# Attention over channels and two expert layers: order of the norms and scores, the product for the merged weights, and weight buffers of the second layer

## The reference

```python
qn = q / (norm(q, axis=1) + 1e-06)        # norms run over the 6016 rows, for each channel
kn = k / (norm(k, axis=1) + 1e-06)
s = kn.transpose(0, 2, 1) @ qn / tau      # 256 x 256
a = exp(s - s.max(-1)); a /= a.sum(-1) + 1e-09
x = v @ a                                 # 6016 x 256
h = x @ moe_w_in                          # 256 x 2048
y = (moe_s * relu(h)**2 + moe_b) @ moe_w_out
h = y @ moe2_w_in
out = (max(h, 0) + moe2_alpha * min(h, 0)) @ moe2_w_out
```

## Time and profile before

| | |
|---|---|
| median of 3 runs | 1071.3 us (1070.34 to 1072.33) |
| the profiled execution | 1070.1 us, span 1068.3 us |
| PE busy | 1032.1 us (97% of the span), 4579 matrix instructions |
| DVE busy | 856.6 us (80%) |
| ACT busy | 607.5 us (57%) |
| POOL busy | 40.9 us (4%) |
| chain that ended last | PE 88%, DVE 4%, DMA 2%, SP's queue 2% |
| moved by DMA | 77.04 MB, mean 72 GB/s |
| mean granted clock of PE | 0.985 of full |

### The profile page before, as it was taken

The page is one execution under the profiler, slowest core; times in us unless marked ns, Lnnn a source line. Parts: engine busy times, 40 slices in busy tenths (PEclk is TensorE's granted clock), DMA queues, the critical chain, the costliest instruction groups (busy, mean ns, idle before and its releaser), DMA issues.

```text
span 1068.3 us, 13360 instructions
## 1 busy us (share of the span) xinstructions
PE 1032.1 (97%) x4579; PEld 862.8 (81%) x4579; DVE 856.6 (80%) x1308; ACT 607.5 (57%) x1014; POOL 40.9 (4%) x61
## 2 busy tenths in 40 slices
PE   8879999999999999999979999999999999999995
PEld 6757888888888888888967788888888888888994
DVE  5888998888788798798879978778777777877874
ACT  5565666566567567566656545445445455455452
POOL 1101100000000000020041000000000000000000
PEclk9988999999999999999989999999999999999998
DMA  9721111310410410510740434104104103100201
GB/s 352 236 43 30 40 21 45 114 20 22 137 20 3 156 18 1 164 31 1 264 122 10 146 114 148 30 1 148 30 1 148 31 1 127 34 1 2 38 1 34
DMA packets 136228, 77.04 MB, mean 72 GB/s; under 512 B 102608, under 2 KB 114912, under 8 KB 135904
## 3 DMA queue, kind: packets, MB, share of 16 engines
q1 hardware_dynamic: 136032, 76.18, 23.9%
q0 software_dynamic: 128, 0.01, 0.0%
HBM read 48.44 MB, written 27.72 MB: 71 GB/s over the span
## 4 chain that ended last, share of the span: by engine, by line
PE 88%; DVE 4%; DMA 2%; SPq 2%; issue 1%; ACT 1%; POOL 0%; DVEq 0%; ACTq 0%
PE acc L428 15%; PE acc L430 15%; PE acc L429 15%; PE hab L428 8%; PE hab L429 8%; PE hab L430 8%; PE hcd L428 6%; PE hcd L430 6%; PE hcd L429 6%; PE acc L500 2%; SPq L301 1%; DMA stage<-in_moe_w_in_dram 1%; DMA qk_raw<-in_k_dram 1%; SPq L316 1%; DVE cb L836 1%
## 5 line engine op out<-in xcount | busy, mean ns | idle before, releaser
L653 ACT ACTIVATE g_hi<-cb 128x512 fp32r<-128x512 f32 (+1 forms) x384 | 233.6, 620 | 237.6 <-DVE cb L851 132.6
L428 PE MATMUL acc<-g_hi,wo_hi 128*128 128x512 f32 (+1 forms) x768 | 296.5, 386 | 0.3 <-DVE g_lo L857 0.3
L429 PE MATMUL acc<-g_lo,wo_hi 128*128 128x512 f32 (+1 forms) x768 | 296.2, 386 | 0.0
L430 PE MATMUL acc<-g_hi,wo_lo 128*128 128x512 f32 (+1 forms) x768 | 296.1, 386 | 0.0
L857 DVE TENSOR_TENSOR g_lo<-cb,g_hi 128x512 fp32r<-128x512 f32 (+1 forms) x384 | 245.3, 679 | 54.0 <-ACT g_hi L653 53.1
L428 PEld LDWEIGHTS acc<-g_hi,wo_hi 128*128 128x128 f32 x768 | 144.4, 188 | 27.6 <-DVE g_lo L857 0.6
L429 PEld LDWEIGHTS acc<-g_lo,wo_hi 128*128 128x128 f32 x768 | 144.5, 188 | 27.1
L430 PEld LDWEIGHTS acc<-g_hi,wo_lo 128*128 128x128 f32 x768 | 144.4, 188 | 27.1
L428 PE MATMUL hab<-x_hi,ws_hi 128*128 128x512 f32 (+1 forms) x384 | 149.5, 389 | 11.3 <-ACT u L635 10.5
L851 DVE SCALAR_TENSOR_TENSOR cb<-cb,alph 128x512 f32<-128x512 f32 (+1 forms) x192 | 142.1, 740 | 20.3 <-ACT cb L635 14.2
L429 PE MATMUL hab<-x_lo,ws_hi 128*128 128x512 f32 (+1 forms) x384 | 148.6, 387 | 0.0
(11 more groups left out here) (121 smaller groups left out, 950.0 us busy)
## 6 DMA issues: line engine op xcount, KB each, us to landing
x_dram<-x_hi SPq DMA_DIRECT2D x35, 256.0 KB, 2.6
x_dram<-x_lo SPq DMA_DIRECT2D x35, 256.0 KB, 2.8
x_hi<-x_dram SPq DMA_DIRECT2D x35, 256.0 KB, 4.8
x_lo<-x_dram SPq DMA_DIRECT2D x35, 256.0 KB, 5.1
qk_raw<-in_q_dram SPq DMA_DIRECT2D x10, 512.0 KB, 10.3
qk_raw<-in_k_dram SPq DMA_DIRECT2D x10, 512.0 KB, 11.5
v_raw<-in_v_dram SPq DMA_DIRECT2D x40, 128.0 KB, 3.3
out_dram<-y_sq SPq DMA_DIRECT2D x80, 64.0 KB, 2.2
```

What stands on the lines that cost most here:

```text
L428: pe.matmul(dst, w_hi, m_hi, start=start, stop=False, skip_group_check=True)
L429: pe.matmul(dst, w_hi, m_lo, start=False, stop=False, skip_group_check=True)
L430: return pe.matmul(dst, w_lo, m_hi, start=False, stop=stop, skip_group_check=True)
L653: sc.activation(g_hi[:, blk, 0:w], cb[:, blk, 0:w], ACT.Copy).then_inc(g_hi_done[blk], 1)
```

## The change

- Chunks of q and k are 1, 2, 2, 3, nine times 4, 2, 1 rows. `sq_sum` is cleared by DVE; a chunk is added by one instruction instead of two; the first fold comes before the last two chunks. PE does six products of ones ahead of the first chunk.
- `scores(i, m)` does one of two channel parts. The last four chunks (11 rows) are done for part 0 first: the first of them ahead of the column sums, the other three behind; then the row of norms; then part 1 of two chunks, turning of part 0 of a, part 1 of the last two chunks. Softmax runs by parts (`soften`, `largest`, `inverse_sum`, `turn_a`, `a_copy`).
- W_in is loaded as fp32 into `win` and not split; a is copied as fp32. A block of merged weights is two fp32 products (`w1_block`, L529 of the changed kernel). Six blocks come ahead of step 0, blocks 6 and 7 within it. Step 0 has an order of its own on ACT and DVE (`first_step`), and its weights are rounded in four parts (`w0_high`, `w0_low`).
- Layer two's weights have six buffers; four lie in `xf`. A step's weights are loaded by two transfers instead of four. The weights of steps 2 to 5 are requested behind `store_x2(4)` and ahead of the reads of x. `ws_at`, `wo_at` prepare layer two's weights at other steps.
- An output tile is stored in four transfers for both channel blocks instead of four for each; two of the last eight are issued by ACT.

The core of the diff:

```diff
 CHUNK = 4
-HEAD_ROWS, TAIL_ROWS = (1, 2), (3, 1)
-ROWS_OF = HEAD_ROWS + (CHUNK,) * ((ROWS - sum(HEAD_ROWS + TAIL_ROWS)) // CHUNK) + TAIL_ROWS
+ROWS_OF = (1, 2, 2, 3) + (CHUNK,) * 9 + (2, 1)
 CHUNKS = len(ROWS_OF)
 ROW_AT = [sum(ROWS_OF[:i]) for i in range(CHUNKS)]
...
-            second = {4: (8, 9), 5: (10, 11), 6: (12, 13), 7: (14,), 8: (15,)}
+            second = {3: (8,), 4: (9, 10), 5: (11, 12), 6: (13,), 7: (14,), 12: (15,)}
...
-            first = (n + 1,) if n + 1 < STEPS else ()
-            second = {4: (8, 9), 5: (10, 11), 6: (12,), 7: (13,), 8: (14,), 9: (15,)}
+            first = (0, 1) if n == 0 else (n + 1,) if n + 1 < STEPS else ()
+            second = {4: (8,), 5: (9, 10), 6: (11, 12), 7: (13,), 12: (14,), 13: (15,)}
...
-                if j >= 2:
-                    sp.wait_ge(ws_split, STEPS + j - 1)
-                for b, h, slot in ((0, 0, A11), (0, 1, S4), (1, 0, A12), (1, 1, A22)):
-                    sp.dma_start(w2_tmp[j % 2][:, slot, :], w2_blocks[b, h, j]).then_inc(w2_loaded[j % 2], 16)
-
...
+                elif j >= W2_BUFS:
+                    sp.wait_ge(ws_split, STEPS + j - W2_BUFS)
+                elif j >= 2:
+                    sp.wait_ge(out_split, PROD * (PAIRS - 1))
+                tmp, loaded = w2_tmp[w2_buf(j)], w2_loaded[w2_buf(j)]
+                sp.dma_start(tmp[:, A11:S4 + 1:S4 - A11, :], w2_blocks[0, j]).then_inc(loaded, 16)
+                sp.dma_start(tmp[:, A12:A22 + 1, :], w2_blocks[1, j]).then_inc(loaded, 16)
...
+            for j in range(2, W2_BUFS):
+                load_w2(j)
             load_x(PAIRS)
-            for i in (2, 4):
-                load_w2(i)
-                load_w2(i + 1)
+            for j in range(W2_BUFS, STEPS):
+                load_w2(j)
+            for i in range(2, STEPS - 1):
                 load_wo(STEPS + i)
-                load_wo(STEPS + i + 1)
-            load_w2(6)
-            load_w2(7)
-            load_wo(STEPS + 6)
-            load_wo(STEPS + 7)
             store_x2(PAIRS - 1)
             load_x(PAIRS + 1)
+            load_wo(2 * STEPS - 1)
...
+                for t in range(2):
+                    store_y(run - 1, t)
+            store_y(RUNS - 1, 0)
+            store_y(RUNS - 1, 1, range(0, G, 2))
...
+            def turn_a(m):
+                pe.wait_ge(exp_done, m + 1)
+                for b in range(CB):
+                    mm = pe.transpose(a_t_ps[m][:, b, :], prob[:, m, b * P:(b + 1) * P], ident[:])
+                mm.then_inc(a_turned, 1)
+
+            def w1_block(i):
+                g, m, h, _slot = W1_BLOCKS[i]
+                pe.wait_ge(a_copied, m + 1)
+                cols = slice((2 * h + g) * WQ, (2 * h + g + 1) * WQ)
+                for b in range(CB):
+                    mm = pe.matmul(w1_banks[i], a_t[:, b, m * P:(m + 1) * P], win[:, b, cols], start=(b == 0), stop=(b == CB - 1))
+                mm.then_inc(w1_ready, 1)
+
...
+            for _ in range(WARM):
+                pe.matmul(h_a[0][:, 0:P], ones[:], ones[:], start=True, stop=True)
+
+            late = CHUNKS - LATE
+            for i in range(late):
+                for m in range(CB):
+                    scores(i, m)
...
+            scores(late, 0)
...
+            for i in range(late + 1, CHUNKS):
+                scores(i, 0)
...
+            for i in range(late, CHUNKS - SHORT):
+                scores(i, 1)
+            turn_a(0)
+            for i in range(CHUNKS - SHORT, CHUNKS):
+                scores(i, 1)
+            pe.wait_ge(win_loaded, 16 * CB)
+            w1_block(0)
+            w1_block(1)
+            w1_block(2)
+            turn_a(1)
+            for i in range(3, 6):
+                w1_block(i)
...
-            for i in range(4):
-                win_high(i)
+            x_high(0, 0)
+            x_high(0, 1)
...
+            soften(0)
+            a_copy(0)
             x_high(0, 2)
-            sc.wait_ge(rsum_ready, 1)
-            w1_copy(0, 0)
-            w1_copy(0, 1)
+            soften(1)
...
+            def first_step():
+                copy(0, 0, m1_done, sum_done[C11], s1, 0, s1_done)
+                w0_high(2)
+                w0_high(3)
+                g_high(0, C11)
+                w1_copy(6)
+                copy(0, 0, m6_done, sum_done[C12], u2, 0, u2_done)
+                w1_copy(7)
+                copy(0, 0, m7_done, sum_done[C22], u3, 1, u3_done)
+                for i in ws_at(0)[:1]:
+                    ws_high(i)
+                for i in wo_at(0)[:1]:
+                    wo_high(i)
+                g_high(0, C22)
+                c21(0, 0)
+                for i in ws_at(0)[1:]:
+                    ws_high(i)
+                for i in wo_at(0)[1:]:
+                    wo_high(i)
+
...
+            def first_step():
+                ve.wait_ge(w1_copied, 6)
+                merge(slice(0, 1))
+                sum_of(0, C11)
+                w0_low(2)
+                gate(0, C11)
+                w0_low(3)
+                g_low(0, C11)
+                merge(slice(1, 4))
+                for i in ws_at(0)[:1]:
+                    ws_low(i)
+                for i in wo_at(0)[:1]:
+                    wo_low(i)
+                sum_of(0, C22)
+                gate(0, C22)
+                g_low(0, C22)
+                for i in ws_at(0)[1:]:
+                    ws_low(i)
+                for i in wo_at(0)[1:]:
+                    wo_low(i)
+
...
+            def fold(half):
+                ve.tensor_tensor(sq_sum[:, :, 0:half, :], sq_sum[:, :, 0:half, :], sq_sum[:, :, half:2 * half, :],
+                                 ALU.add).then_inc(squares_added, 1)
```

More of the change, by code:

```diff
@@ L89, in out_squares @@
         at = token(pair, t)
-        return out[at:at + width(pair)].rearrange("(a j) (b g c) -> b g a j c", a=SQ, b=CB, c=SQ)
+        return out[at:at + width(pair)].rearrange("(a j) (b g c) -> g a (j b) c", a=SQ, b=CB, c=SQ)
     with ExitStack() as ctx:
@@ L181, in build @@
         qk_loaded = [sem(f"qk_loaded{i}") for i in range(RAW)]
-        win_loaded = [sem(f"win_loaded{b}") for b in range(CB)]
+        win_loaded = sem("win_loaded")
         v_loaded = sem("v_loaded")
@@ L437, in product @@
                     pe.wait_ge(x_loaded[run % 2], 16 * 2 * PROD * ((run - PAIRS) // 2 + 1))
-                if s == A11 and run % PAIRS == 0:
-                    pe.wait_ge(ws_split, layer(run) * STEPS + j + 1)
+                if run == 0 and j == 0:
+                    pe.wait_ge(w0_split, next(i for i, (a, b) in enumerate(W0_PARTS) if a <= s < b) + 1)
+                elif s == A11 and run % PAIRS == 0:
+                    pe.wait_ge(ws_split, layer(run) * STEPS + j)
                 return three_passes(dst[:, 0:w], ws_hi[:, j, s, :], ws_lo[:, j, s, :],
@@ L585, in x_high @@
                 if i == 0 and run == 1:
-                    sc.wait_ge(ws_split, STEPS)
+                    sc.wait_ge(ws_split, STEPS - 1)
+                if i == 0 and run == 0:
+                    sc.wait_ge(consts_ready, 4)
                 sc.wait_ge(v_turned, 2 * CB * run + (2, 2, 4)[min(i, 2)])
@@ L693, in step @@
                 splits(run, j, 1)
-                if j == 0 and run > 0:
+                if j == 0:
                     for b in range(CB):
@@ L873, in turn_y @@
                     ve.wait_ge(out_split, PROD * PAIRS)
-                wait(ve, y_stored, 16 * G * 4 * (run - PAIRS))
-                ve.transpose(by_squares(y_sq[:, CB * t + b, 0:width(run)]), by_squares(src)).then_inc(y_turned, 1)
+                wait(ve, y_stored, 16 * G * 2 * (run - PAIRS))
+                ve.transpose(y_sq[:, t, b:width(run) // SQ * CB:CB, :], by_squares(src)).then_inc(y_turned, 1)
             def middle(run, j):
@@ L934, in _ @@
                 ve.wait_ge(squares_done, i + 1)
-                wait(ve, squares_added, i)
-                for a in range(2):
-                    last = ve.tensor_tensor(sq_sum[:, a, 0:r, :], sq_sum[:, a, 0:r, :], sq[:, i % 2, a, 0:r, :], ALU.add)
-                last.then_inc(squares_added, 1)
-            for n, half in enumerate((CHUNK // 2, CHUNK // 4)):
-                ve.wait_ge(squares_added, CHUNKS + n)
-                ve.tensor_tensor(sq_sum[:, :, 0:half, :], sq_sum[:, :, 0:half, :], sq_sum[:, :, half:2 * half, :],
-                                 ALU.add).then_inc(squares_added, 1)
```

285 lines of the change are left out of this document (136 added, 149 removed).

## The result

The changed kernel takes 1061.8 us (median of 4 runs, 1059.1 to 1064.7) against 1071.2 us, a ratio of 0.991 (95% interval 0.988 to 0.994). The forecast was 1053.4, its range ended at 1059.5. The profiled execution took 1059.1 us (span 1057.3), 11.0 us less than the one of before and less than the other three executions; it is the one in which the clock fell least.

What follows compares the result with a forecast made beforehand. PE's work plus its stands and low-clock time was taken as the bound. Gains of 1.9 (front), 11 (change of layers) and 4.4 (tail) sum to 17.3 us, giving 1052.8 or 1054.0, middle 1053.4 us; range 1048.8 to 1059.5.

Steps and rivals of the forecast that it cites:

- the term for the change of layers: Between layers one and two: earlier weight requests remove PE's 6.4 us stand and its low clock, gaining 11 us (8.5 to 11.8).
- the 0.8: Change of layers: 0.5 and 0.3 us set against the gain, for fuller step 5 and steps 4 and 5 of layer two.
- its rival: Change of layers: output weights come late in step 5, half the stand returns; 5.5 us gained instead of 11, 1058.9; 12%.
- The 11.8 us to be had: Around the change of layers, 520 to 600 us: PE's loss counted from missing products, 9.0 + 0.6 + 2.2 us.
- The load of step 5: Step 5, change of layers: two weights and two output weights, 4.1 us of DVE where 2.9 are free; costs PE 0.5.
- The front: Scores through steps 0 and 1: gains 1.9 us if the clock drops near 42 us, 4.7 without.
- from there PE and DVE keep the distance: After step 1's C22 sum: PE (10.2 us a step) and DVE (10.1) keep the lead gained, 4.7 us before any clock drop.
- the fall behind step 0: Front, at 74 us: a second clock drop hides under 5 us of waits of step 1.
- The single steps: Front times: stand 2.3 us before the column sums, root 44.5, merged weights from 52.4, step 0 at 63.2, C22 sum 88.9.
- both branches: Front: clock drops at the stand before the column sums (forecast, 1053.4, 45%) or does not (rival, 1050.6, 30%).
- The tail: Last tile pair's stores: eight of double size, two issued by ACT, instead of sixteen; gains 4.4 us.

Runs made afterwards that it cites:

- the first edit: Weights 10 rounded in step 5 instead of 4, weights 12 in step 6 instead of 5, against the unedited changed kernel: 1064.1 us.

## Why the prediction was wrong, step by step

**The step that failed is the term for the change of layers**, 11 us, measured 3.7. The missing 7.3 us have three parts, of 5.0, 1.4 and 1.7 us, less the 0.8 which the prediction had set for a load that did not show in this kernel:

- The prediction had all four weights merged by 531 and named no time at which ACT wants weights 10; the 537 of its rival is for the output weights. The table takes weights 10 in step 4, where ACT comes to them at 522.4, and they were merged at 525.1. That is 3.3 us of PE, and with the stand came the low clock the prediction had removed with it: 3.4 us at half speed, 1.7 more. The request time was right (517.5, right behind the stores); what was never held against it was the time at which the moved rounding would ask. The edit that takes weights 10 a step later removed this stand. A request cost 0.69 us and not 0.48, eight of them 5.6 us instead of 4, which adds to it.
- Output weights 10 came late in step 5: 1.4 us. The prediction had this as a rival with 12%, at a price of 5.5 us, and argued that they are wanted by 537 and requested by 533. Both times were about right (537.7 and 533.9); but behind the reads of x the transfer took 5.3 us. The mechanism was real; the first edit shows its full price once the stand ahead of it is gone, 6.7 us.
- The 11.8 us to be had were counted too high by 1.7. Added up from the trace of before, PE's idle time from 520 to 620 is 8.5 us and the low clock costs 1.6, 10.1 in all: the clock fell at 541.3 for 6.8 us, but PE stood through the first 3.5 of them.

```profile
541.30:544.83 3.53, 0.00 (x1) 0.00 (x1) 2.20 (x5) 2.97 (x6) 0.47 (x1) 0.50 0.26 74
```

The same sum over the trace of after is 6.6 (4.95 and 1.7), so 3.5 were gained by it, 3.7 by the lead. The count of products in windows, on which the 11.8 rested, gives more than PE lost.

The load of step 5, set at 0.5 us, is a fourth error, hidden here behind the waits. With the waits for transfers gone it was 1.6 in step 5 and 2.0 in step 6, partly since POOL's merges now run beside DVE: three `g_low` took 2.5 us instead of 1.7.

**The front**: 1.9 with a fall of the clock, 4.7 without. At the C22 sum of step 1, where the prediction stopped its working, the lead was 5.1 and 4.5 in the two profiled executions of this kernel, both without the fall at 42, and 1.1 to 1.9 in the five kernels with the same front and the fall. So up to there it was right within 0.8 us. Measured in runs 1 to 4 it is 3.0 to 3.7 and -0.4 to 0.4. What failed is the sentence that from there PE and DVE keep the distance: the clock fell once more behind step 1, at 89 to 93, and that took 1.4 to 1.5 us in each of these executions. The prediction had seen only the fall behind step 0, and rightly put it at nothing. With the fall at 42 go 2.6 to 4.1 us, not 2.8, and up to 1.4 of them are the late chunk itself. The single steps held: stand 2.1 (2.3), root 44.1 (44.5), blocks at 51.6 (52.4), step 0 at 61.7 (63.2), the C22 sum of step 1 at 88.3 (88.9). What the prediction did not see is that both branches belong to one kernel: it gave 45% and 30% to two kinds of program, and one or the other came from execution to execution, in the traces with the landing of a chunk. The Trainium skill (TensorE: Matmul & The Clock Gate, the section on HAM oscillation), cited in the prediction, spoke for no fall. The traces show one behind stands of 2.5 and 3.0 us too, which are shorter than the page asks for; the measurement decides.

**The tail**: 4.4 forecast, 4.3 measured. Issues took 0.8 us instead of 0.66, the stores moved 187 GB/s instead of the 172 estimated, and the end came 7.6 us after PE (7.5 to 8 forecast). That the sum came out to 0.1 us is in part luck: the first error is for the worse, the second for the better.

**The drift**: each of the last four steps of run 11 takes 0.17 us more than before, 0.7 in all, with no stand. It occurs in the profiles of several kernels and not in others; its cause is open.

The sum for a typical execution: front between 0 and 3.7, change of layers 3.7, tail 4.3, less up to 0.7, gives 7 to 12; the median gained 9.4.

## What to carry to other kernels

When a wait is removed, find the time at which each engine behind it will ask for its next input, and hold that against the time at which the input is there; here two inputs were late one behind the other, and mending one made the kernel slower. Asking for the data earlier gave 3.7 us. Asking for them where they are already there, and spreading the work evenly on the engine that has least slack, made it 8.8, of which the even load is some 2.3. Add up idle time and time at the low clock from the trace rather than count products in windows. And a stand ahead of a short chain is worth filling, even with products of ones, when it is long enough in some executions for the clock to fall.

## What the runs showed of the hardware

- After over 20 us of work without a gap, stands of PE of 2.5 to 3.6 us (five traces) were followed by 6.8 us at 1.2 GHz, stands of 2.1 us (two traces) were not. Products of ones, one in 0.22 us, in most of the stand kept the clock at 2.4 GHz in all six traces with them, also where 0.9 us of it stayed empty.
- What a fall costs depends on who ends the step: 1.4 to 1.5 us for 3.4 us at 1.2 GHz behind step 1, nothing behind step 0, where DVE is last.
- One chunk of q and k landed 0.3 to 1.4 us late in ten of the thirteen profiled executions since the change, always at about the same place of the stream (23 to 26 us). The one trace of the kernel before does not show it, and has no stand that it could have lengthened.
- POOL and DVE slow each other when both work on SBUF: DVE by 37% on subtractions of two SBUF tiles, by 11% on the gate, not at all on sums out of PSUM; POOL by 50%.
